# Centroid similarities of clustered attention, computed with tokens on the partitions

## What is computed

```python
# q, k, v: (2, 8, 768, 64); centroids: (8, 16, 64)
q_assign = argmax(einsum('bhsd,hcd->bhsc', q_n, c_n), axis=-1)   # q_n, k_n, c_n: normalised
k_assign = argmax(einsum('bhsd,hcd->bhsc', k_n, c_n), axis=-1)
mask = q_assign[:, :, :, None] == k_assign[:, :, None, :]
scores = where(mask, scale * q @ k.T, -1e9)
attn = softmax(scores) ; attn_out = attn @ v
x = moe(attn_out) ; out = (x @ w_a * (x @ w_b)) @ w_out
```

## Time and profile before

| | |
|---|---|
| three executions | 966.73, 971.63, 979.37 us; median 971.63 |
| profiled execution | 973.64 us, of which 971.8 us are the span of instructions |
| 0 to 60 us: first heads | TensorE clock granted: 0.72 of full |
| 60 to 340 us: rounds 0 to 12 | TensorE busy 258.5 of 280 us, VectorE 224.8, GpSimd 160.7, ScalarE 100.8 |
| 340 to 410 us: last rounds, router | |
| 410 to 972 us: experts and feed-forward | TensorE busy 519.5 of 562 us |

### The profile page before, as it was taken

One profiled execution on the slowest core, in us unless ns is written; L12 is line 12 of the kernel. 1 busy time (PEld: TensorE's weight loads), 2 busy tenths in 40 slices (PEclk: granted clock), 3 DMA queues, 4 the chain that ended last, 5 costly groups with the idle time before them and its releaser, 6 DMA issues.

```text
span 971.8 us, 11830 instructions
## 1 busy us (share of the span) xinstructions
PE 880.1 (91%) x4205; PEld 620.6 (64%) x4206; DVE 513.0 (53%) x683; ACT 293.4 (30%) x558; POOL 225.8 (23%) x175
## 2 busy tenths in 40 slices
PE   5799989999899989509999999969999999999998
PEld 2455555555445554207777777757888888888886
DVE  4667888777888755626566665534321311131111
ACT  3133333333333334503434444423121211121111
POOL 6045655655665442150000000020000100000000
PEclk9579999988999989858999999988999999999999
DMA  4122222222221121366555555652000200010001
GB/s 123 50 70 67 71 68 75 73 78 72 75 67 48 48 82 60 140 222 237 199 199 204 202 196 206 211 183 74 0 1 1 87 1 1 0 44 1 1 1 43
DMA packets 41105, 86.93 MB, mean 89 GB/s; under 512 B 4216, under 2 KB 10584, under 8 KB 41056
## 3 DMA queue, kind: packets, MB, share of 16 engines
q1 hardware_dynamic: 39136, 79.99, 25.4%
q0 software_dynamic: 1920, 6.29, 1.9%
HBM read 60.53 MB, written 17.83 MB: 81 GB/s over the span
## 4 chain that ended last, share of the span: by engine, by line
PE 80%; DVE 11%; issue 6%; DMA 1%; ACT 0%; SPq 0%; DVEq 0%; POOL 0%; ACTq 0%
PE bank L1414 7%; PE bank L1415 7%; PE bank L1416 7%; PE bank L1214 4%; PE pair L1161 4%; PE bank L1354 3%; PE first_pair L1345 3%; PE first_pair L1346 3%; PE first_pair L1347 3%; PE bank L1355 3%; PE bank L1356 3%; PE first_pair L1199 3%; PE first_pair L1201 3%; DVE has_tmp L890 2%; PE bank L1131 2%
## 5 line engine op out<-in xcount | busy, mean ns | idle before, releaser
L1088 DVE TENSOR_TENSOR g_sb<-bank,a_sb 128x512 f32<-128x512 f32 x36 | 24.9, 692 | 196.7 <-PE bank L1416 196.7
L1414 PE MATMUL bank<-x_hi,wt 128*128 128x512 f32 x288 | 115.0, 399 | 1.4 <-DVE x_lo L1057 1.4
L1415 PE MATMUL bank<-x_lo,wt 128*128 128x512 f32 x288 | 114.6, 398 | 0.0
L1416 PE MATMUL bank<-x_hi,wt 128*128 128x512 f32 x288 | 114.5, 398 | 0.0
L844 DVE TENSOR_REDUCE neg_max<-pair 128x1 f32<-128x768 f32 x93 | 88.5, 951 | 45.8 <-PE pair L1161 45.7
L346 POOL TENSOR_TENSOR prob_sum<-prob_sum,prob 128x768 f32<-128x768 f32 x56 | 102.5, 1831 | 11.6 <-ACT prob L582 9.6
L959 DVE TENSOR_TENSOR wt<-w_raw,wt 128x2048 fp32r<-128x2048 f32 x41 | 92.9, 2287 | 10.2 <-ACT wt L661 9.8
L582 ACT ACTIVATE prob<-first_pair 128x384 f32<-128x384 f32 x128 | 59.6, 486 | 83.7 <-PE first_pair L1201 56.6
L1214 PE MATMUL bank<-prob,v_sb 128*64 128x384 f32 x384 | 83.8, 520 | 0.0
L1161 PE MATMUL pair<-kc,qb 96*128 96x384 f32 x186 | 61.7, 417 | 6.1 <-DVE neg_max L844 5.2
L1414 PEld LDWEIGHTS bank<-x_hi,wt 128*128 128x128 f32 x288 | 54.6, 190 | 15.1 <-DVE x_lo L1057 1.8
(11 more groups left out here) (212 smaller groups left out, 1666.1 us busy)
## 6 DMA issues: line engine op xcount, KB each, us to landing
w_raw<-in_moe_w_dram SPq DMA_DIRECT2D x32, 1024.0 KB, 5.2
x_slots<-zeros SPq DMA_DIRECT2D x10, 512.0 KB, 3.7
x_slot<-x_slots SPq DMA_DIRECT2D x18, 256.0 KB, 4.0
y_slots<-y_sb SPq DMA_DIRECT2D x16, 256.0 KB, 4.5
q_raw<-in_q_dram SPq DMA_DIRECT2D x16, 192.0 KB, 2.4
k_raw<-in_k_dram SPq DMA_DIRECT2D x16, 192.0 KB, 2.5
v_sb<-in_v_dram SPq DMA_DIRECT2D x16, 192.0 KB, 2.3
qb<-qa SPq DMA_DIRECT2D x16, 192.0 KB, 2.6
```

What stands on the lines that cost most here:

```text
L1414: pe.matmul(to[:, :], w[0], x2_hi[:, kk, :], start=(kk == 0), stop=False)
L1415: pe.matmul(to[:, :], w[0], x2_lo[:, kk, :], start=False, stop=False)
L1416: last = pe.matmul(to[:, :], w[1], x2_hi[:, kk, :], start=False, stop=(kk == KD - 1))
```

## The change

Units 4, 5 and 6 become one unit 4. For each of the six token tiles and for q and k, the operand tile (128 x 128, float32r) is the stationary operand, and `cn_split` moves: 32 columns, 16 of the centroids rounded to float32r and 16 of what is left. So 12 matmuls write tokens to the partitions at once, with two numbers for each similarity. ScalarE's two copies, `logit_sb` and the six transposes are gone. In `one_hot` a new first step on VectorE, `tensor_reduce` with add, sums the two numbers, 128 x 384 in PSUM to 128 x 192 in SBUF (`logit_sum`); the bank is free after it. `lmax` and `eq` read `logit_sum` in SBUF in place of the bank. Later units are numbered 5 and 6, and a head has 7 steps in place of 9. Two VectorE instructions at the start make `cn_split` from `cn_t`.

```diff
         cn_t = sba("cn_t", [P, H, C], F32)
+        cn_split = sba("cn_split", [P, H, 2 * C], F32R)
...
-        logit_sb = sba("logit_sb", [3 * C, S], F32)
+        logit_sum = sba("logit_sum", [P, 2 * NT, C], F32)
...
-            return t0, t0_full, t0_free, 9 * (n - (n > 1))
+            return t0, t0_full, t0_free, 7 * (n - (n > 1))
...
# ScalarE
-                for unit in (4, 5):
-                    for n in made(r): unit0(n, unit)
-                    if r == 0 and unit == 4: row_max(1)
+                if r == 0: row_max(1)
...
# VectorE, centroids_in
-                dve.tensor_copy(cn_t[:], bank[0][:, 0:P].rearrange("p (h c) -> p h c", h=H))
+                link(dve.tensor_copy(cn_t[:], bank[0][:, 0:P].rearrange("p (h c) -> p h c", h=H)))
+                link(dve.tensor_copy(cn_split[:, :, 0:C], cn_t[:]))
+                dve.tensor_tensor(cn_split[:, :, C:2 * C], cn_t[:], cn_split[:, :, 0:C].bitcast(F32), ALU.subtract)
...
# VectorE, one_hot
-                lg = at[:, 0:3 * NT * C].rearrange("p (t g c) -> p t g c", g=3, c=C)[:, :, 0:3:2, :]
+                lg = at[:, 0:4 * NT * C].rearrange("p (t l c) -> p t c l", l=2, c=C)
...
-                dve.wait_ge(full, base + 7)
-                link(dve.tensor_reduce(lmax[:].rearrange("p (t g) -> p t g", g=2), lg, AX.X, ALU.max))
-                dve.tensor_tensor(eq[:].rearrange("p (t g) c -> p t g c", g=2), lg,
-                                  lmax[:].rearrange("p (t g) -> p t g", g=2)[:, :, :, None].to_broadcast([P, NT, 2, C]),
-                                  ALU.is_equal).then_inc(free, 1)
-                dve.wait_ge(free, base + 7)
+                dve.wait_ge(full, base + 5)
+                dve.tensor_reduce(logit_sum[:], lg, AX.X, ALU.add).then_inc(free, 1)
+                dve.wait_ge(free, base + 5)
+                link(dve.tensor_reduce(lmax[:], logit_sum[:], AX.X, ALU.max))
+                link(dve.tensor_tensor(eq[:], logit_sum[:], lmax[:, :, None].to_broadcast([P, 2 * NT, C]),
+                                       ALU.is_equal))
...
# TensorE, unit0
-                elif unit < 6:
-                    cols = slice((unit - 4) * HALF, (unit - 3) * HALF)
-                    for row, src in ((0, qa), (32, kd)):
-                        last = pe.matmul(at[row:row + C, 0:HALF], cn_t[:, h, :], src[u][:, cols].bitcast(F32),
-                                         start=True, stop=True)
-                elif unit == 6:
+                elif unit == 4:
                     for t in range(NT):
-                        last = pe.transpose(at[:, t * 3 * C:(t + 1) * 3 * C], logits_of[0:3 * C, t * P:(t + 1) * P],
-                                            cst[0:3 * C, C_ID:C_ID + 3 * C])
+                        for g, src in ((0, qa), (1, kd)):
+                            last = pe.matmul(at[:, (2 * t + g) * 2 * C:(2 * t + g + 1) * 2 * C],
+                                             src[u][:, t * P:(t + 1) * P], cn_split[:, h, :], start=True, stop=True)
...
# TensorE, the order in a round
                 for n in masked(r)[:1]: masked_scores(n, 2)
                 for n in made(r): unit0(n, 4)
                 if s_: times_v(r, 2)
                 for n in masked(r)[:1]: masked_scores(n, 3)
-                for n in made(r): unit0(n, 5)
                 if s_: times_v(r, 3)
                 for n in masked(r)[:1]: masked_scores(n, 4)
                 if s_: scores_t(r, 5)
-                for n in made(r): unit0(n, 6)
                 if s_: times_v(r, 4)
```

More of the change, by code:

```diff
@@ L385, in hot_rows @@
                 free, base = operand_bank(n)[2:]
-                sp.wait_ge(free, base + 8)
+                sp.wait_ge(free, base + 6)
                 sp.dma_start(qb[u][D:D + C, :].bitcast(F32), hot_t[s][0:C, :].bitcast(F32)).then_inc(ops_in[u], 16)
@@ L587, in unit0 @@
                 at, full, free, base = operand_bank(n)
-                logits_to = prob_sum if n == 1 else logit_sb
                 act.wait_ge(full, base + unit + 1)
@@ L591, in unit0 @@
                     act.wait_ge(st_full, 12 * (n - 4) + 12)
[L592 to L597, removed]
+                to = (qa if unit < 2 else kd)[u][:, (unit % 2) * HALF:(unit % 2 + 1) * HALF]
+                ins = act.activation(to, at[:, 0:HALF], ACT.Copy)
                 ins.then_inc(free, 1)
@@ L867, in mask_rows @@
                 at, full, free, base = operand_bank(n)
-                dve.wait_ge(full, base + 8)
+                dve.wait_ge(full, base + 6)
                 if n >= 2:
@@ L885, in find_keys @@
                 at, full, free, base = operand_bank(n)
-                dve.wait_ge(full, base + 9)
+                dve.wait_ge(full, base + 7)
                 dve.wait_ge(hot_ready, n + 1)
                 dve.tensor_scalar(has_key[:], at[:, 0:C], 0.5, None, ALU.is_gt).then_inc(free, 1)
-                dve.wait_ge(free, base + 9)
+                dve.wait_ge(free, base + 7)
                 link(dve.tensor_tensor(has_tmp[:], hot[s][:, :, 0:C],
@@ L1121, in unit0 @@
                 at, full, free, base = operand_bank(n)
-                logits_of = prob_sum if n == 1 else logit_sb
                 if base + unit > 0:
@@ L1131, in unit0 @@
                         last = pe.transpose(at[:, i * P:(i + 1) * P], src[:, t, :].bitcast(F32), ident)
-                elif unit < 6:
-                    cols = slice((unit - 4) * HALF, (unit - 3) * HALF)
-                    for row, src in ((0, qa), (32, kd)):
-                        last = pe.matmul(at[row:row + C, 0:HALF], cn_t[:, h, :], src[u][:, cols].bitcast(F32),
-                                         start=True, stop=True)
-                elif unit == 6:
+                elif unit == 4:
                     for t in range(NT):
-                        last = pe.transpose(at[:, t * 3 * C:(t + 1) * 3 * C], logits_of[0:3 * C, t * P:(t + 1) * P],
-                                            cst[0:3 * C, C_ID:C_ID + 3 * C])
-                elif unit == 7:
+                        for g, src in ((0, qa), (1, kd)):
+                            last = pe.matmul(at[:, (2 * t + g) * 2 * C:(2 * t + g + 1) * 2 * C],
+                                             src[u][:, t * P:(t + 1) * P], cn_split[:, h, :], start=True, stop=True)
+                elif unit == 5:
                     pe.wait_ge(hot_ready, n + 1)
@@ L1209, in times_v @@
                     if n == 0:
-                        pe.wait_ge(second_free, 9)
+                        pe.wait_ge(second_free, 7)
                     if n >= 1:
@@ L1245, in _ @@
                 if r == 0: masked_scores(1, 2)
-                for n in masked(r)[:1]: unit0(n, 7)
+                for n in masked(r)[:1]: unit0(n, 5)
                 if s_: scores_t(r, 1)
@@ L1255, in _ @@
                 if p4: unit1("sum", r - 1)
-                for n in masked(r)[:1]: unit0(n, 8)
+                for n in masked(r)[:1]: unit0(n, 6)
                 if s_: times_v(r, 0)
@@ L1263, in _ @@
                 for n in masked(r)[:1]: masked_scores(n, 0)
-                if r == -2: unit0(1, 7)
+                if r == -2: unit0(1, 5)
                 if p4: unit1("out", r - 1)
@@ L1269, in _ @@
                 for n in masked(r)[:1]: masked_scores(n, 1)
-                if r == -2: unit0(1, 8)
+                if r == -2: unit0(1, 6)
                 for t in early_tile(r, 1): turn_x(t, pair[:, t % 2, :])
```

## The result

The changed kernel takes 978.01 us (median of 20 runs, 974.81 to 990.52) against 970.96 us for the kernel before (20 runs on the same chips, 965.01 to 979.37): a ratio of 1.0093 with a 95% interval of 1.0075 to 1.0112. It is 0.9% slower. The ratio is that of the fast runs and leaves out the one of 990.52 us; the two medians by themselves are 7.05 us apart, 0.7%. The profiled execution took 974.81 us, its span 973.0.

A forecast was written before the change was run, and what follows sets the result against it. At the full clock the loop runs over GpSimd and the port it shares with VectorE. 9.4 + 1.4 - 1.6 = +9.2 us on 973.64 gives 982.8, against the median 980.8, stated as 981; 8-in-10 range 957 to 992.

The forecast's parts named there:

- What bounds the kernel: Full-clock round of 21.16 us: the loop runs over GpSimd and the port shared with VectorE, not the removed TensorE work.
- TensorE's saving at nothing: Units 4 to 6: TensorE is won 0.8 us a head, covered by waits for `k_split` and `hot`, so no gain.
- Rival (d): New unit 4: the narrow matmuls are slow, 2.3 us a head, price hidden; 981 to 983 us; chance 0.04.
- Rival (a): Whole round: TensorE is the bound after all and the chain through `hot` gives way; 960 us; chance 0.22.
- The length of the sum: New first step of `one_hot`: taken as 0.82 us like `v_sum`, with 0.56 and 1.35 as ends.
- rival (b): `one_hot`: sum of 0.56 us, `eq` slips through, `eqd` waits, `hot` +0.67 in 9 rounds; 975.5 us; chance 0.18.
- +1.04 in nine rounds: `one_hot` at full clock: `eq` waits for GpSimd's addition, `hot` ends 1.04 us later; 9 rounds give +9.4 us.
- The four rounds of before: Rounds where `eqd` already waits: `hot` ends +0.36 later if `eq` loses, 0 if it wins; counted as +1.4 us.
- The start: Before the steady rounds: `cn_split` costs 1.0, head 0 gains 1.4, head 2 0.2; together -1.6 us, bounds -3 and +2.
- Rival (c): TensorE's clock falls more often: one more low stretch in 9 rounds costs 9 us; 990 or more; chance 0.13.

The follow-up runs named there:

- e2: Changed kernel with only the 16 rounded centroid columns moved, so there is no sum; similarities less exact: 966.69 us, ratio 0.9975.
- e1: Kernel before plus one VectorE copy of the logits from PSUM to SBUF, read by `lmax` and `eq`: 981.34 us, ratio 1.0119.
- e3: Changed kernel with `desc` and `lmax` in spare PSUM columns from head 2 on: 953.89 us, ratio 0.9832 against the kernel before.
- e4: Kernel before with `desc` in PSUM for `eqd` and `hot`: 968.99 us, ratio 0.9979.
- second repeat: A further profile of a kernel, unedited, after its first profile and one repeat: 964.30 us for the kernel before, 979.63 us for the changed one.
- e5: e3 with `has_key` in PSUM as well and `lost` computed by GpSimd: 927.76 us, ratio 0.9596 against the kernel before.
- e7: Kernel before, old units 4 to 6 kept, with `desc` and the keys in PSUM and `lost` on GpSimd: 935.97 us, ratio 0.9674.
- e6: e5 with the casts of q and k on ScalarE in place of VectorE: 922.16 us, ratio 0.9530 against the kernel before.

## Why the prediction was right, and where it was not

The forecast was 981, 1% slower; measured was a ratio of 1.0093, which on the 971.63 it started from is 980.7 (978.7 by the two medians). What bounds the kernel was right. The duration of the new sum was not, so another step waited than the forecast said, and two further terms lay off in the other direction.

**What bounds the kernel.** "At the full clock the loop runs over GpSimd and the port that it shares with VectorE, not over the TensorE work that the change removes" was shown from both sides: e2 keeps the saving without the added step and stays at 21.17; e1 has the added step without the saving and goes to 21.94; e3 removes the port wait by the place of an operand and goes to 20.54. That TensorE stood only 0.12 us behind (e4) I had not seen; I had given it "room" by the wait of 0.51 at L1161.

**TensorE's saving at nothing.** Right: 12 pairs take 1.40 to 1.51 us from first start to last end where 1.3 was predicted, so a round is spared 0.66 us of TensorE's time and not 0.8, and masked scores 4 wait 0.66 us for row maxima 3 where it was 0.51: what is saved is waited there and before the transposes of `hot`. Rival (d) falls with the pairs at 0.114 each. Rival (a), 960, is decided against by e2. It needed `v_fill` to come earlier in the round, and `v_fill` follows a chain that starts at the transposes of `hot`.

**The length of the sum: the step that failed.** "I take 0.82, the same operation on the same count" came out at 0.548 (13 executions). The straight line through the PSUM reads of 192 and 768 elements gave 0.56. I had preferred `v_sum` as the only strided sum; what makes that one longer by 0.27 us does not come with results or with pairs 64 bytes apart in PSUM. The Trainium skill (VectorE: DVE Perf Modes, The perf-mode tier table), with one element per cycle for `tensor_reduce` from any memory, agrees with the 0.548; its caution on consecutive elements (Advanced Engine Details and Errata, PSUM Cachelines) shows nothing here. The step decided more than 0.27 us of hidden time. It decided which step meets the closed port.

**So the rounds went as rival (b).** `eq` slipped through in 11 of 13 rounds, `eqd` waited, "hot ends at 180.79, +0.67": measured +0.69 a round. My forecast had +1.04 in nine rounds, with `eq` waiting 1.9 us in them; in none of these did `eq` wait so. The two rounds of 13 in which it waited (1.56) end in the transposes of heads 3 and 15, and there `eqd` had waited before. In place of the 1.04, 0.69 came in 11 rounds, those with a low stretch too (with one such stretch they took 22.1 to 22.6 before and 22.8 to 23.5 after), where I had +0.36 and rival (b) none: 7.6 us in place of 9.4 + 1.4 = 10.8. The four rounds of before in which `eqd` waited already I took as fixed. They are not: in both repeats `eqd` waits for heads 3 and 15 alone, and at the end of the other rounds, with a single low stretch or none, it is `hot`; the other two of the first profile come at the end of its two rounds with twice as much low clock (23.97 and 23.98 us).

**The start.** Predicted -1.6 with bounds of -3 and +2. Against the first profile it is -3.3 (71.82 to 68.48), against the two repeats +0.5 on average. The clock goes with the difference: in the first profile of before it was low from 26.3 to 60.4 us, in the second repeat from 23.9 to 51.1 but for 3.3 us, in the changed kernel from 16.9 to 51.0. The first profile had half the clock earlier too, which its record of the granted clock does not show: that record reads full up to 26 us, while the matmuls of L1135 from 17.2 to 21.6 take 0.82 to 0.85 us, against 0.49 at 20.7 in the second repeat, at the full clock. So the 0.72 that stands for the first 60 us of the kernel before is too high. The logits of head 0 do come earlier. In the second repeat of the kernel before the timeline has

```profile
21.77 0.36 DVE L854 TENSOR_REDUCE lmax<-bank 128x12 f32<-128x192 f32 x1 [5.06 <-PE bank L1139]
```

and in the changed kernel

```profile
20.82 0.56 DVE L850 TENSOR_REDUCE logit_sum<-bank 128x192 f32<-128x384 f32 x1 [2.83 <-PE bank L1130]
```

with `lmax` at 21.41. That is 1.76 earlier than in the first profile (23.17), from which I forecast 1.4, but only 0.36 earlier than in the repeat, in which the clock rose before the matmuls were through. One profile was not enough to size this term.

**Low stretches.** Rival (c) had "one more low stretch in 9 rounds", 9 us more. They went from 3 to 5 of 11 rounds to 7, their cost from 6.4 to 8.8 us. The direction was right, the size a quarter. The profile of before that I worked from held more of this than the repeats do (9.3 against 6.0 and 3.8 us), so its base already had part of what the rival would add.

**Why the number still came out.** Rounds 3.2 less than predicted, start 0.8 more, low stretches 2.4 more, which the forecast did not have: -3.2 + 0.8 + 2.4 = 0. The agreement within 1 us is a cancellation, luck and not accuracy; and the last two terms rest on three profiles of each kernel, among which the low stretches of before alone differ by 5.5 us.

**What stays open** is what sets when the clock falls. Of 11 rounds 3 to 5 had a low stretch at 21.16 us, 7 at 21.85; in e3 none came from 100 to 322 us, in e5 and e7 none from about 50 to 338, in e6 none from 67 to 354. The length of the round does not order the cases: e1, with rounds of 21.94, had low stretches in 8 of 11, but so had e4 with 21.04, and e2 with 21.17 in 3. Nor does the time in it in which TensorE is not busy: 1.9 us in e4 and in the kernel before, 2.0 in e3, 2.6 in e2, 2.7 in e1, 3.3 in the changed kernel. No run varied it by itself.

## What to carry to other kernels

An instruction that lasted 1.5 us in one place and 0.3 in another, on the same shapes and with its operands in the same memory, was waiting here; no view of waits showed it. List durations by form, look at minimum and maximum, and see whose work ends where the long ones end. A step added to a chain that runs beside another engine's long instructions is priced by which of the later steps it pushes into them, not by its own length; take those steps off the shared port first (one input in PSUM, tiny steps on the other engine, casts on a third), and only then remove work from the engine that is busy 90% of the time.

## What the hardware showed that was not expected

- A sum over pairs 64 bytes apart in PSUM (384 f32 elements to 192 results) took 0.548 us, as a dense read would by the line through the earlier trace rows; a sum of as many elements in SBUF with 64 results took 0.82.
- A `tensor_scalar` on six numbers per partition lasts until GpSimd's addition ends: 0.17 us free, 1.53 beside it. Taking it off VectorE was part of the 1.5 us a round between e3 and e5.
- Reductions ran beside GpSimd's additions at their free length each time (`dmax` 0.35 at 178.26 in the kernel before, with an addition from 178.08; the sum 0.55 at 221.97 in the changed one, with an addition from 221.30).
- Pairs of a 128 column weight load and a 32 column matmul follow one another at 0.114 us at 2.4 GHz, below the 0.19 of a single load as the trace records it.
- In e6, where TensorE waits least, no stretch at 1.2 GHz lies between 67 and 354 us. Its record of the granted clock reads full before that as well, but a matmul of 384 columns (L1207) takes 0.53 us at 43.9 and 0.34 at 66.8: the first heads ran at half the clock there as in the other versions, and the record begins too late to show it.
